# Waits for attention and for the next unit's bank moved ahead of the last feed-forward matmuls

## Chip, cores and metric

One core of one Trainium2 chip. The metric is device time in microseconds (us) of one execution; the median over several executions is compared.

## What is computed

Three stages follow each other on 4 x 576 tokens of width 512 (8 heads of 64). The parts that matter here, cut from the reference:

```python
# 1: windowed attention; heads 0-3 see 32 keys back, heads 4-7 see every 4th of 128
scores = np.where(masks, scale * q @ k.T, -1e9)
attn = softmax(scores) @ v
# 2: token-shifted feed-forward
xk = mu_k * x + (1 - mu_k) * x_prev ; xr = mu_r * x + (1 - mu_r) * x_prev
k = np.maximum(xk @ w_k, 0.0)
x = sigmoid(xr @ w_r) * (k * k @ w_v)
# 3: low-rank mix over tokens, then a second feed-forward
u = x + (x.T @ U @ V).T
out = u + np.maximum(u @ w_ch1, 0.0) @ w_ch2
```

## The kernel before, in words

It is written by hand: each engine has its own program, and the order of work on an engine is the order of its text. Engines wait for each other with counting semaphores; the helper `wait` (L366) puts a wait in front of the next instruction of the engine. TensorE (PE) runs its queue in order, so everything behind an unmet wait stands still.

**Feed-forward units.** Stage 2 goes over the tokens in 9 chunks of 256 (`NC1`, the PE function `chunk`, L1274). A chunk has 10 units in the order of `UNITS` (L148): eight "k" units (one 128-column block of `xk @ w_k`) and two "r" units (`xr @ w_r`). A unit is 4 steps over the contraction, each a call of `three` (L1185), which issues three fp32r matmuls (high x high, low x high, high x low), so 12 matmuls: 256 moving columns in a k unit, 512 in an r unit. Units alternate between two PSUM banks (`unit_bank`). ScalarE (ACT) empties a bank (`relu_k`, L843, or `sig`, L849) and counts `unit_out`; before writing, unit n waits until unit n-2 was emptied. After some units come the matmuls of `k*k @ w_v` for the blocks named in `V_AFTER` (L149), six of 512 columns for each block; these wait for `sql_done`, which VectorE (DVE) counts at L1050.

**Attention visits.** Attention of the tokens that later chunks need is woven in between. It works on 32 pieces (8 parts k of the tokens times 4 pairs of heads p), each in four steps: A transposes q and k, B makes scores, C transposes the probabilities, D multiplies with v. `SLOT_OF` gives each step a place behind one of the 10 units; what stands behind a unit is called its visit here. From chunk 1 on the visits behind units 0, 3, 5 and 8 hold an A and a C step, those behind units 1, 4, 6 and 9 a B and a D step; units 2 and 7 have none. On PE `other_work` (L1245) runs them: after the unit and its w_v matmuls, except behind unit 9, where the visit stands ahead of these. The A steps and C steps are transposes (L1203, L1205, L1232), the B and D steps small matmuls into 64-column halves of the array (L1226, L1241).

Every step writes one or two of four banks that are used in turn. In `attention` (L1191) PE waits, bank by bank, until the bank's last use was emptied; A also waits for its q and k loads, B until its A was copied out, C for the normalised probabilities (`normed`, DVE L1023), D for its v load and until its C was copied out. ACT copies C's banks out at L733 (`probs_t`), in the order of its own program: after the unit's relu and square, the first half of the exponentials of the B step in the visit before (L743), then A's `q_t` copy (L724), then `probs_t`. Its counter is `att_scalar`, that of DVE's copies `att_vector`.

```python
                    if GROUP[key] >= ABANKS:
                        wait_drained(pe, GROUPS[GROUP[key] - ABANKS])
                    ...
                        pe.wait_ge(values_in[n % VALUES], V_COUNT[n])
                        wait_drained(pe, last_bank("C", k, p))
```

Chunks 7 and 8 carry the token mix of stage 3 in place of attention; from 418 us on the second feed-forward runs alone.

Of the kernel before, what the change touches and what calls it, by code (L numbers as in the profile page):

```python
# [30 lines left out]
D = H * DH  # L31
# [8 lines left out]
KT = D // P  # L40
# [54 lines left out]
def steps_in(slot):  # L95
    return sorted([step for step, n in SLOT_OF.items() if n == slot], key=lambda step: ("ACBD".index(step[0]), step[1:]))
# [26 lines left out]
def last_bank(st, k, p):  # L123
    return (st, k, p, banks_of((st, k, p)) - 1)
# [84 lines left out]
def build(nc, q, k_in, v, mu_k, mu_r, w_k, w_v, w_r, u_in, v_in, w_ch1, w_ch2, out):  # L209
    ctx = ExitStack()  # L210
    with ctx:
# [159 lines left out]
        def wait(eng, s, value):  # L371

            value = value + CREDIT.get(id(s), 0)
            if isinstance(value, int) and value <= 0:
                return
            eng.wait_ge(s, value)

        def wait_drained(eng, key):

            n = GROUP[key]  # L380
            if drained_by_scalar(key):
                wait(eng, att_scalar, SCALAR_N[n])
            else:
                wait(eng, att_vector, VECTOR_N[n])

        def wait_mm(eng, key):

# [794 lines left out]
        def _(pe):  # L1182
            pe.sem_inc(o_mm, CREDIT[id(o_mm)])

            def three(dst, lhs, rhs, start, stop):  # L1185
# [2 lines left out]
                pe.matmul(dst, lhs[0], rhs[1], start=False, stop=False)  # L1188
                return pe.matmul(dst, lhs[1], rhs[0], start=False, stop=stop)  # L1189

            def attention(stage_, k, p):  # L1191
                n, dil, half = nth(k, p), DILATED[p], k % 2
                for j in range(banks_of((stage_, k, p))):
                    key = (stage_, k, p, j)
                    dst = abank(key)
                    if GROUP[key] >= ABANKS:
                        wait_drained(pe, GROUPS[GROUP[key] - ABANKS])
                    if stage_ == "A":
                        if j == 0:
                            pe.wait_ge(qk_in[n % RAWS], QK_COUNT[n])  # L1200
                        raw = (q_raw, k_raw)[j][n % RAWS]
                        for t in range(2):
                            ins = pe.transpose(dst[:, t * P:t * P + P], raw[:, t, :], ident[:, :])  # L1203
                        if half:
                            ins = pe.transpose(dst[:, WHOLE:WHOLE + TAIL], raw[0:TAIL, 2, :], ident[0:TAIL, 0:TAIL])  # L1205
                    elif stage_ == "B":
                        if j == 0:
                            wait_drained(pe, ("A", k, p, 0))
                            wait_drained(pe, ("A", k, p, 1))
                        every = units(k, p)  # L1210
                        for i, (query, col, keys) in enumerate(every):
                            if (i == DILATION and dil) != (j == 1):
                                continue
                            if not dil:
                                rhs = k_t[p][:, FROM[half] + UQ * i:FROM[half] + UQ * i + keys]
                            elif keys == 2 * UK:
                                rhs = k_t[p][:, 0:S].rearrange("p (r j) -> p r j", r=DILATION)[:, :, SUB - UK // 2:SUB]
                            else:
                                first_key = SUB * i + (JCUT - WINDOW if half else 0)
                                rhs = k_t[p][:, first_key:first_key + keys]  # L1220
                            col -= every[DILATION][1] if j else 0
                            for h in range(2):
                                out_ = dst[DH * h:DH * h + DH, col:col + keys]
                                if keys == 2 * UK:
                                    out_ = out_.rearrange("p (r j) -> p r j", r=DILATION)
                                ins = pe.matmul(out_, q_t[n % 2][:, h, query:query + UQ], rhs, start=True, stop=True)  # L1226
                    elif stage_ == "C":
                        if j == 0:
                            wait(pe, normed, n + 1)
                        cols = [(col + UK * a, min(keys, UK)) for _, col, keys in units(k, p) for a in range(max(1, keys // UK))]  # L1230
                        for i, (col, keys) in enumerate(cols[4 * j:4 * j + 4]):
                            ins = pe.transpose(dst[0:keys, i * P:i * P + P], probs[n % 2][:, col:col + keys], ident[:, :])  # L1232
                    else:
                        pe.wait_ge(values_in[n % VALUES], V_COUNT[n])
                        wait_drained(pe, last_bank("C", k, p))
                        for i, (query, _, keys) in enumerate(units(k, p)):
                            blocks = max(1, keys // UK)
                            for a in range(blocks):
                                for h in range(2):
                                    rows, kk = slice(DH * h, DH * h + DH), min(keys, UK)  # L1240
                                    ins = pe.matmul(dst[rows, query:query + UQ], v_raw[n % VALUES][0:kk, i + a, rows],  # L1241
                                                    probs_t[n % 2][0:kk, i + a, rows], start=a == 0, stop=a == blocks - 1)
                    ins.then_inc(att_mm, 1)

            def other_work(c, n):  # L1245

                if c < MIX_CHUNK:
                    for step in steps_in(c * NUNIT + n):
                        attention(*step)
                else:  # L1250
                    for step in mix_steps("tensor", [(c - MIX_CHUNK) * NUNIT + n]):
                        mix_step(*step)

            def turn(c, t):
# [16 lines left out]
                                       x[:, n, t * P:t * P + P] if start else u_tile[:, t, n * P:n * P + P], ident[:, :])  # L1271
                ins.then_inc(t_mm, 1)

            def chunk(c):  # L1274
                last = c == NC1 - 1
                for n, (kind, m) in enumerate(UNITS):
                    wait(pe, unit_out, c * NUNIT + n - 1)
                    dst = unit_bank[n % 2]
                    if kind == "k":
                        if m == 0:  # L1280
                            wait(pe, xkl_done, c + 1)
                        if c == 0 and m % 2 == 0:
                            pe.wait_ge(w_split, SPLIT1["k", m // 2])
                        cols = slice((m % 2) * P, (m % 2) * P + P)
                        for t in range(KT):
                            ins = three(dst[:, 0:C1], (wk_h[:, m // 2, t, cols], wk_l[:, m // 2, t, cols]),
                                        (xs_h[:, 0, t, :], xs_l[:, 0, t, :]), t == 0, t == KT - 1)
                    else:
                        if m == 0:
                            wait(pe, xrl_done, c + 1)  # L1290
                        if c == 0 and m == 0:
                            pe.wait_ge(w_split, SPLIT1["r", 1])
                        cols = slice(m * P, m * P + P)
                        for t in range(KT):
                            ins = three(dst[:, :], (xs_h[:, 1, t, cols], xs_l[:, 1, t, cols]),
                                        (wr_h[:, t, :], wr_l[:, t, :]), t == 0, t == KT - 1)
                    ins.then_inc(unit_mm, 1)
                    if last and n == NUNIT - 1:
                        for t in range(T2):
                            turn(0, t)  # L1300
                    if n == NUNIT - 1:
                        other_work(c, n)
                    for m2 in V_AFTER[n]:
                        if m2 == 0:
                            wait(pe, x2_done, c * T1)
                        if c == 0 and m2 % 2 == 0:
                            pe.wait_ge(w_split, SPLIT1["v", m2 // 2])
                        wait(pe, sql_done, c * M1 + m2 + 1)
                        for t in range(T1):
                            cols = slice(t * P, t * P + P)  # L1310
                            ins = three(v_bank[t][:, :], (sq_h[:, m2 % KRING, cols], sq_l[:, m2 % KRING, cols]),
                                        (wv_h[:, m2, :], wv_l[:, m2, :]), m2 == 0, m2 == M1 - 1)
                        ins.then_inc(v_mm, 1)
                    if n < NUNIT - 1:
                        other_work(c, n)
# [35 lines left out]
            pe.wait_ge(consts, 1)  # L1351
            pe.wait_ge(cleared, 3)
            for step in BEFORE:
                attention(*step)
            for c in range(NC1):
                chunk(c)
# [65 lines left out]
```

## Time and profile before

| | |
|---|---|
| time, median of 3 | 834.91 us (834.12 to 838.01) |
| profiled execution: its own time | 836.28 us |
| its span, first to last instruction | 834.5 us |
| PE busy in the span | 794.1 us (95%) |
| DVE busy | 323.6 us (39%) |
| ACT busy | 332.2 us (40%) |
| GpSimd (POOL) busy | 152.1 us (18%) |
| mean granted PE clock | 0.977 |

The profile is one execution. The timeline gives start and duration of each instruction, equal ones merged. PE's durations are modelled and overlap, so the distance between two starts says how long a matmul holds the engine. "PEld" is the weight load of a matmul. A bracket at a row's end is the engine's idle time before it and what ended it; the list of waits sums these up.

### The profile page before, as it was taken

What the parts mean: (1) busy time and instruction counts of PE and PEld (TensorE: products, weight loads), DVE (VectorE), ACT (ScalarE), POOL (GpSimd) and SP (SyncE); (2) the same over time, 40 slices, a digit from 0 to 9 for tenths busy, and PEclk for the clock granted to TensorE, in tenths of its full rate; (3) what the DMA queues carried; (4) which work ended last, traced back from release to release, by engine and by line L of the source; (5) the groups of instructions that cost most, each with busy time, mean ns of one, the idle gap of its engine ahead of it and who ended that gap; (6) DMA issues with size and microseconds to landing.
All of it is one profiled execution on the core that took longest, in us unless ns stands there. A gap on an engine that the chain in (4) does not pass through costs nothing.

```text
span 834.5 us, 13588 instructions
## 1 busy us (share of the span) xinstructions
PE 794.1 (95%) x5176; PEld 695.9 (83%) x5176; DVE 323.6 (39%) x660; ACT 332.2 (40%) x885; POOL 152.1 (18%) x169
## 2 busy tenths in 40 slices
PE   5579999989999999989999999999999999999998
PEld 4357888878888888877889899999989999999997
DVE  5556846464647463673541131121122113113111
ACT  5558676767676765552343211111111111111110
POOL 5694201030102012330056500000000000000000
PEclk8679999999999999998999999999999999999999
DMA  5544231023212200100023210000000000001001
GB/s 130 145 125 114 63 82 45 14 74 83 55 42 59 55 14 1 51 7 20 1 95 132 77 39 1 1 25 12 0 0 38 0 0 38 0 0 38 1 0 38
DMA packets 83349, 35.78 MB, mean 43 GB/s; under 512 B 71136, under 2 KB 77280, under 8 KB 83296
## 3 DMA queue, kind: packets, MB, share of 16 engines
q1 hardware_dynamic: 83296, 35.07, 15.3%
q8 instruction: 33, 0.54, 0.3%
q14 instruction: 20, 0.16, 0.1%
HBM read 30.33 MB, written 4.72 MB: 42 GB/s over the span
## 4 chain that ended last, share of the span: by engine, by line
PE 86%; DVE 4%; ACT 3%; POOL 2%; SPq 2%; issue 1%; DMA 1%; DVEq 0%; ACTq 0%; POOLq 0%
PE bank L1187 25%; PE bank L1189 25%; PE bank L1188 25%; PE bank L1226 3%; PE bank L1232 2%; PE bank L1241 2%; PE bank L1203 2%; SPq L449 1%; PE bank L1270 1%; DMA k_raw<-in_k_dram 1%; PE bank L1205 1%; DVE sq L1046 1%; PE bank L1329 1%; ACT probs L743 1%; POOL wr_l L622 1%
## 5 line engine op out<-in xcount | busy, mean ns | idle before, releaser
L925 ACT ACTIVATE h_h<-bank 128x384 fp32r<-128x384 f32 x96 | 47.2, 492 | 332.2 <-PE bank L1189 332.2
L1157 DVE SCALAR_TENSOR_TENSOR h_l<-bank,h_h 128x384 fp32r<-128x384 f32 x96 | 53.5, 557 | 308.9 <-ACT h_h L925 308.9
L1187 PE MATMUL bank<-ut_h,w_h 128*128 128x384 f32 x384 | 130.4, 340 | 0.0
L1189 PE MATMUL bank<-ut_h,w_l 128*128 128x384 f32 x384 | 129.3, 337 | 0.0
L1188 PE MATMUL bank<-ut_l,w_h 128*128 128x384 f32 x384 | 128.9, 336 | 0.0
L1189 PE MATMUL bank<-w_h,h_l 128*128 128x512 f32 x288 | 113.8, 395 | 0.0
L1188 PE MATMUL bank<-w_l,h_h 128*128 128x512 f32 x288 | 113.6, 394 | 0.0
L1187 PE MATMUL bank<-w_h,h_h 128*128 128x512 f32 x288 | 112.0, 389 | 0.0
L1187 PE MATMUL bank<-xs_h,wk_h 128*128 128x256 f32 x288 | 85.9, 298 | 0.7 <-DVE xs_l L1116 0.7
L1188 PE MATMUL bank<-xs_l,wk_h 128*128 128x256 f32 x288 | 81.6, 283 | 0.0
L1189 PE MATMUL bank<-xs_h,wk_l 128*128 128x256 f32 x288 | 81.4, 283 | 0.0
L1187 PEld LDWEIGHTS bank<-ut_h,w_h 128*128 128x128 f32 x384 | 72.2, 188 | 3.1
L1188 PEld LDWEIGHTS bank<-ut_l,w_h 128*128 128x128 f32 x384 | 72.2, 188 | 3.1
L1189 PEld LDWEIGHTS bank<-ut_h,w_l 128*128 128x128 f32 x384 | 72.1, 188 | 0.0
L843 ACT ACTIVATE relu_k<-bank 128x256 f32<-128x256 f32 x72 | 27.2, 377 | 102.4 <-PE bank L1189 101.8
L1187 PE MATMUL bank<-wv_h,sq_h 128*128 128x512 f32 x144 | 58.9, 409 | 6.1 <-DVE sq_l L1050 6.1
L1189 PEld LDWEIGHTS bank<-w_h,h_l 128*128 128x128 f32 x288 | 54.0, 188 | 11.5
L1188 PEld LDWEIGHTS bank<-w_l,h_h 128*128 128x128 f32 x288 | 54.0, 188 | 9.4
L1187 PEld LDWEIGHTS bank<-w_h,h_h 128*128 128x128 f32 x288 | 54.1, 188 | 8.9
L1187 PEld LDWEIGHTS bank<-xs_h,wk_h 128*128 128x128 f32 x288 | 55.4, 192 | 4.6 <-DVE xs_l L1116 1.4
L1188 PE MATMUL bank<-wv_l,sq_h 128*128 128x512 f32 x144 | 57.4, 399 | 0.0
L1189 PE MATMUL bank<-wv_h,sq_l 128*128 128x512 f32 x144 | 57.4, 399 | 0.0
(126 smaller groups left out, 1341.3 us busy)
## 6 DMA issues: line engine op xcount, KB each, us to landing
stage<-in_moe_w_ch_dram SPq DMA_DIRECT2D x16, 512.0 KB, 3.3
out_dram<-result SPq DMA_DIRECT2D x18, 256.0 KB, 2.0
q_raw<-in_q_dram SPq DMA_DIRECT2D x64, 64.0 KB, 2.2
k_raw<-in_k_dram SPq DMA_DIRECT2D x64, 64.0 KB, 2.2
v_raw<-in_v_dram SPq DMA_DIRECT2D x32, 64.0 KB, 2.3
stage<-in_moe_w_k_dram SPq DMA_DIRECT2D x4, 512.0 KB, 4.2
stage<-in_moe_w_v_dram SPq DMA_DIRECT2D x4, 512.0 KB, 3.8
v_raw<-in_v_dram SPq DMA_DIRECT2D x16, 96.0 KB, 2.6
```

The costliest lines, as they stand in the source:

```text
L449: sp.dma_start(dst[:, 0:2, DH * h:DH * h + DH], rows.rearrange("(t p) d -> p t d", p=P)).then_inc(landed, 16)
L622: ins = pool.tensor_tensor(lo[:, a], raw[:, a], hi[:, a].bitcast(F32), ALU.subtract)
L843: act.activation(relu_k[:, m % 2, :], unit_bank[n % 2][:, 0:C1], ACT.Relu).then_inc(unit_out, 1)
L925: act.activation(h_h[:, m % KRING, :], h_bank[m % 2][:, 0:C2], ACT.Relu).then_inc(hh_done, 1)
L1157: dve.scalar_tensor_tensor(h_l[:, m % KRING, :], h_bank[m % 2][:, 0:C2], 0.0, h_h[:, m % KRING, :].bitcast(F32), op0=ALU.max, op1=ALU.subt ...
L1187: pe.matmul(dst, lhs[0], rhs[0], start=start, stop=False)
L1188: pe.matmul(dst, lhs[0], rhs[1], start=False, stop=False)
L1189: return pe.matmul(dst, lhs[1], rhs[0], start=False, stop=stop)
L1203: ins = pe.transpose(dst[:, t * P:t * P + P], raw[:, t, :], ident[:, :])
L1226: ins = pe.matmul(out_, q_t[n % 2][:, h, query:query + UQ], rhs, start=True, stop=True)
L1232: ins = pe.transpose(dst[0:keys, i * P:i * P + P], probs[n % 2][:, col:col + keys], ident[:, :])
L1241: ins = pe.matmul(dst[rows, query:query + UQ], v_raw[n % VALUES][0:kk, i + a, rows], probs_t[n % 2][0:kk, i + a, rows], start=a == 0, stop ...
```

## The change

`attention` on PE loses all its waits. The new `attention_waits` issues, for all steps of a visit together, the waits for their banks, loads, copies and normalised probabilities. In the part before the chunks and in chunk 0 it is called right ahead of each step. In chunks 1 to 6 the new `ahead` calls it inside the unit, before the fourth call of `three`, or, where w_v matmuls stand between the unit and its visit, before the last call of `three` of those. `ahead` also takes the wait for `unit_out` that the next unit needs to the same place, in all nine chunks. No compute instruction is added, taken away or put elsewhere.

```diff
@@ -383,6 +383,15 @@
             else:
                 wait(eng, att_vector, VECTOR_N[n])
 
+        def wait_all_drained(eng, keys):
+
+            by_scalar = [SCALAR_N[GROUP[key]] for key in keys if drained_by_scalar(key)]
+            by_vector = [VECTOR_N[GROUP[key]] for key in keys if not drained_by_scalar(key)]
+            if by_scalar:
+                wait(eng, att_scalar, max(by_scalar))
+            if by_vector:
+                wait(eng, att_vector, max(by_vector))
+
         def wait_mm(eng, key):
 
             wait(eng, att_mm, GROUP[key] + 1)
@@ -1188,25 +1197,34 @@
                 pe.matmul(dst, lhs[0], rhs[1], start=False, stop=False)
                 return pe.matmul(dst, lhs[1], rhs[0], start=False, stop=stop)
 
+            def attention_waits(steps):
+
+                keys = [GROUPS[GROUP[st, k, p, j] - ABANKS] for st, k, p in steps for j in range(banks_of((st, k, p)))
+                        if GROUP[st, k, p, j] >= ABANKS]
+                keys += [("A", k, p, j) for st, k, p in steps if st == "B" for j in range(2)]
+                keys += [last_bank("C", k, p) for st, k, p in steps if st == "D"]
+                wait_all_drained(pe, keys)
+                for st, k, p in steps:
+                    n = nth(k, p)
+                    if st == "A":
+                        pe.wait_ge(qk_in[n % RAWS], QK_COUNT[n])
+                    elif st == "C":
+                        wait(pe, normed, n + 1)
+                    elif st == "D":
+                        pe.wait_ge(values_in[n % VALUES], V_COUNT[n])
+
             def attention(stage_, k, p):
                 n, dil, half = nth(k, p), DILATED[p], k % 2
                 for j in range(banks_of((stage_, k, p))):
                     key = (stage_, k, p, j)
                     dst = abank(key)
-                    if GROUP[key] >= ABANKS:
-                        wait_drained(pe, GROUPS[GROUP[key] - ABANKS])
                     if stage_ == "A":
-                        if j == 0:
-                            pe.wait_ge(qk_in[n % RAWS], QK_COUNT[n])
                         raw = (q_raw, k_raw)[j][n % RAWS]
                         for t in range(2):
                             ins = pe.transpose(dst[:, t * P:t * P + P], raw[:, t, :], ident[:, :])
                         if half:
                             ins = pe.transpose(dst[:, WHOLE:WHOLE + TAIL], raw[0:TAIL, 2, :], ident[0:TAIL, 0:TAIL])
                     elif stage_ == "B":
-                        if j == 0:
-                            wait_drained(pe, ("A", k, p, 0))
-                            wait_drained(pe, ("A", k, p, 1))
                         every = units(k, p)
                         for i, (query, col, keys) in enumerate(every):
                             if (i == DILATION and dil) != (j == 1):
@@ -1225,14 +1243,10 @@
                                     out_ = out_.rearrange("p (r j) -> p r j", r=DILATION)
                                 ins = pe.matmul(out_, q_t[n % 2][:, h, query:query + UQ], rhs, start=True, stop=True)
                     elif stage_ == "C":
-                        if j == 0:
-                            wait(pe, normed, n + 1)
                         cols = [(col + UK * a, min(keys, UK)) for _, col, keys in units(k, p) for a in range(max(1, keys // UK))]
                         for i, (col, keys) in enumerate(cols[4 * j:4 * j + 4]):
                             ins = pe.transpose(dst[0:keys, i * P:i * P + P], probs[n % 2][:, col:col + keys], ident[:, :])
                     else:
-                        pe.wait_ge(values_in[n % VALUES], V_COUNT[n])
-                        wait_drained(pe, last_bank("C", k, p))
                         for i, (query, _, keys) in enumerate(units(k, p)):
                             blocks = max(1, keys // UK)
                             for a in range(blocks):
@@ -1246,6 +1260,8 @@
 
                 if c < MIX_CHUNK:
                     for step in steps_in(c * NUNIT + n):
+                        if c == 0:
+                            attention_waits([step])
                         attention(*step)
                 else:
                     for step in mix_steps("tensor", [(c - MIX_CHUNK) * NUNIT + n]):
@@ -1271,10 +1287,19 @@
                                        x[:, n, t * P:t * P + P] if start else u_tile[:, t, n * P:n * P + P], ident[:, :])
                 ins.then_inc(t_mm, 1)
 
+            def ahead(c, n):
+
+                if 1 <= c < MIX_CHUNK and steps_in(c * NUNIT + n):
+                    attention_waits(steps_in(c * NUNIT + n))
+                if n < NUNIT - 1:
+                    wait(pe, unit_out, c * NUNIT + n)
+
             def chunk(c):
                 last = c == NC1 - 1
                 for n, (kind, m) in enumerate(UNITS):
-                    wait(pe, unit_out, c * NUNIT + n - 1)
+                    visit_after_unit = n == NUNIT - 1 or not V_AFTER[n]
+                    if n == 0:
+                        wait(pe, unit_out, c * NUNIT - 1)
                     dst = unit_bank[n % 2]
                     if kind == "k":
                         if m == 0:
@@ -1283,6 +1308,8 @@
                             pe.wait_ge(w_split, SPLIT1["k", m // 2])
                         cols = slice((m % 2) * P, (m % 2) * P + P)
                         for t in range(KT):
+                            if t == KT - 1 and visit_after_unit:
+                                ahead(c, n)
                             ins = three(dst[:, 0:C1], (wk_h[:, m // 2, t, cols], wk_l[:, m // 2, t, cols]),
                                         (xs_h[:, 0, t, :], xs_l[:, 0, t, :]), t == 0, t == KT - 1)
                     else:
@@ -1292,6 +1319,8 @@
                             pe.wait_ge(w_split, SPLIT1["r", 1])
                         cols = slice(m * P, m * P + P)
                         for t in range(KT):
+                            if t == KT - 1 and visit_after_unit:
+                                ahead(c, n)
                             ins = three(dst[:, :], (xs_h[:, 1, t, cols], xs_l[:, 1, t, cols]),
                                         (wr_h[:, t, :], wr_l[:, t, :]), t == 0, t == KT - 1)
                     ins.then_inc(unit_mm, 1)
@@ -1308,6 +1337,8 @@
                         wait(pe, sql_done, c * M1 + m2 + 1)
                         for t in range(T1):
                             cols = slice(t * P, t * P + P)
+                            if t == T1 - 1 and m2 == V_AFTER[n][-1] and not visit_after_unit:
+                                ahead(c, n)
                             ins = three(v_bank[t][:, :], (sq_h[:, m2 % KRING, cols], sq_l[:, m2 % KRING, cols]),
                                         (wv_h[:, m2, :], wv_l[:, m2, :]), m2 == 0, m2 == M1 - 1)
                         ins.then_inc(v_mm, 1)
@@ -1351,6 +1382,7 @@
             pe.wait_ge(consts, 1)
             pe.wait_ge(cleared, 3)
             for step in BEFORE:
+                attention_waits([step])
                 attention(*step)
             for c in range(NC1):
                 chunk(c)
```

Two places show how the waits move on PE, in chunk 5. Lines L1187 to L1189 of before are L1196 to L1198 of the change, and L1226 and L1241 are L1244 and L1255. Names of semaphores stand behind "waits".

First, unit 1 and its visit, a B and a D step, before:

```order
L1187 MATMUL bank1<-xs_h,wk_h 128x256
L1188 MATMUL bank1<-xs_l,wk_h 128x256
L1189 MATMUL bank1<-xs_h,wk_l 128x256
L1226 MATMUL bank4<-k_t3,q_t1 64x96 [waits att_vector,att_scalar]
L1226 MATMUL bank4<-k_t3,q_t1 64x96 x7
L1241 MATMUL bank5<-probs_t1,v_raw1 64x64 [waits att_scalar,values_in1]
L1241 MATMUL bank5<-probs_t1,v_raw1 64x64 x7
L1187 MATMUL bank0<-xs_h,wk_h 128x256 [waits unit_out]
```

and with the change:

```order
L1196 MATMUL bank1<-xs_h,wk_h 128x256 [waits values_in1,unit_out,att_vector,att_scalar]
L1197 MATMUL bank1<-xs_l,wk_h 128x256
L1198 MATMUL bank1<-xs_h,wk_l 128x256
L1244 MATMUL bank4<-k_t3,q_t1 64x96 x8
L1255 MATMUL bank5<-probs_t1,v_raw1 64x64 x8
L1196 MATMUL bank0<-xs_h,wk_h 128x256
```

All waits of the visit (v load, both copies) and that of unit 2 for its bank now stand three matmuls ahead of the visit; the B and D steps and unit 2 begin without a wait.

Second, the w_v matmuls behind unit 5 and the visit with an A and a C step, before:

```order
L1187 MATMUL bank3<-wv_h,sq_h 128x512
L1188 MATMUL bank3<-wv_l,sq_h 128x512
L1189 MATMUL bank3<-wv_h,sq_l 128x512
L1203 MATMUL bank4<-ident,q_raw2 128x128 [waits qk_in2,att_scalar]
L1203 MATMUL bank4<-ident,q_raw2 128x128
L1205 MATMUL bank4<-ident,q_raw2 128x64
L1203 MATMUL bank5<-ident,k_raw2 128x128 [waits att_vector]
L1203 MATMUL bank5<-ident,k_raw2 128x128
L1205 MATMUL bank5<-ident,k_raw2 128x64
L1232 MATMUL bank6<-ident,probs1 96x128 [waits normed,att_vector]
L1232 MATMUL bank6<-ident,probs1 96x128 x3
L1187 MATMUL bank0<-xs_h,wk_h 128x256 [waits unit_out]
```

and with the change:

```order
L1196 MATMUL bank3<-wv_h,sq_h 128x512 [waits normed,qk_in2,unit_out,att_vector,att_scalar]
L1197 MATMUL bank3<-wv_l,sq_h 128x512
L1198 MATMUL bank3<-wv_h,sq_l 128x512
L1224 MATMUL bank4<-ident,q_raw2 128x128 x2
L1226 MATMUL bank4<-ident,q_raw2 128x64
L1224 MATMUL bank5<-ident,k_raw2 128x128 x2
L1226 MATMUL bank5<-ident,k_raw2 128x64
L1248 MATMUL bank6<-ident,probs1 96x128 x4
L1196 MATMUL bank0<-xs_h,wk_h 128x256
```

The wait for `normed`, which stood ahead of the C step's first transpose, is now ahead of the last three w_v matmuls, together with the load's and the banks'. Where no w_v matmuls follow a unit, as with units 1, 6 and 9, the waits stand inside the unit as in the first place.

## Rows read from the trace of the kernel before

**Rows 1.** Waits of PE, 95.2 to 336.6 us: total, times, longest.

```profile
PE bank L1187 <- DVE sq_l L1050: 2.2, 5, 0.8
PE bank L1203 <- DMA k_raw<-in_k_dram: 1.4, 1, 1.4
```

**Rows 2.** Waits of PE, 95.2 to 420 us (all chunks from 1 on).

```profile
PE bank L1187 <- DVE sq_l L1050: 5.8, 6, 3.7
```

**Rows 3.** Waits of ACT, 95.2 to 336.6 us.

```profile
ACT relu_k L843 <- PE bank L1189: 62.2, 16, 6.5
```

**Rows 4.** Timeline of PE: start, us, instruction; where hoisted waits will stand.

```profile
243.96 0.28 PE L1187 MATMUL bank<-xs_h,wk_h 128*128 128x256 f32 x1
...
253.60 0.28 PE L1187 MATMUL bank<-xs_h,wk_h 128*128 128x256 f32 x1
...
263.61 0.28 PE L1187 MATMUL bank<-xs_h,wk_h 128*128 128x256 f32 x1
...
280.99 0.40 PE L1187 MATMUL bank<-wv_h,sq_h 128*128 128x512 f32 x1
...
284.31 0.28 PE L1187 MATMUL bank<-xs_h,wk_h 128*128 128x256 f32 x1
...
294.93 0.28 PE L1187 MATMUL bank<-xs_h,wk_h 128*128 128x256 f32 x1
...
306.25 0.28 PE L1187 MATMUL bank<-xs_h,wk_h 128*128 128x256 f32 x1
...
306.69 0.55 PE L1226 MATMUL bank<-k_t,q_t 128*64 128x96 f32 x8
...
339.09 0.28 PE L1187 MATMUL bank<-xs_h,wk_h 128*128 128x256 f32 x1
```

**Rows 5.** Timeline of ACT: the C step's copies for the six visits.

```profile
244.31 0.76 ACT L733 ACTIVATE probs_t<-bank 96x512 f32<-96x512 f32 x2
...
253.52 0.59 ACT L733 ACTIVATE probs_t<-bank 64x512 f32<-64x512 f32 x1
...
264.11 0.59 ACT L733 ACTIVATE probs_t<-bank 64x512 f32<-64x512 f32 x1
...
284.38 0.59 ACT L733 ACTIVATE probs_t<-bank 96x512 f32<-96x512 f32 x1
...
295.12 0.86 ACT L733 ACTIVATE probs_t<-bank 96x512 f32<-96x512 f32 x2
...
305.95 0.87 ACT L733 ACTIVATE probs_t<-bank 96x512 f32<-96x512 f32 x2
```

**Rows 6.** Timeline of DVE: the normalising that C waits for, chunk 5.

```profile
280.53 0.56 DVE L1023 TENSOR_TENSOR probs<-probs,inv 128x384 f32<-128x384 f32 x1
```

**Rows 7.** Timeline of ACT: the relu that frees a unit bank, chunk 7.

```profile
338.24 0.39 ACT L843 ACTIVATE relu_k<-bank 128x256 f32<-128x256 f32 x1 [2.87 <-PE bank L1189]
```

**Rows 8.** Timeline of PE: the visit in chunk 3 whose load is late.

```profile
180.24 0.41 PE L1203 MATMUL bank<-ident,q_raw 128*128 128x128 f32 x2 [1.44 <-DMA k_raw<-in_k_dram]
```

**Rows 9.** Timeline of PE: first matmuls after a wait that was not met.

```profile
300.50 0.50 PE L1187 MATMUL bank<-wv_h,sq_h 128*128 128x512 f32 x1 [0.39 <-DVE sq_l L1050]
300.84 0.39 PE L1188 MATMUL bank<-wv_l,sq_h 128*128 128x512 f32 x1
301.07 0.40 PE L1189 MATMUL bank<-wv_h,sq_l 128*128 128x512 f32 x1
```

**Rows 10.** Timeline of PE: unit 3 begins behind two met waits.

```profile
309.77 0.29 PE L1189 MATMUL bank<-xs_h,wk_l 128*128 128x256 f32 x1
309.89 0.40 PE L1187 MATMUL bank<-wr_h,xs_h 128*128 128x512 f32 x1
```

**Rows 11.** Timeline of PEld: load of a 64-row transpose, no wait.

```profile
303.72 0.14 PEld L1205 LDWEIGHTS bank<-ident,q_raw 64*128 64x128 f32 x1 [0.16 <-issue]
```

**Rows 12.** Timeline of PE: unit 2 begins behind a D step.

```profile
308.36 0.39 PE L1187 MATMUL bank<-xs_h,wk_h 128*128 128x256 f32 x1
308.59 0.28 PE L1188 MATMUL bank<-xs_l,wk_h 128*128 128x256 f32 x1
```

## The prediction

> **What bounds the kernel now.** I read the share of busy time first: PE works 794 of 834.5 us (95%, in the table above), no other engine passes 40%. So anything that makes PE stand still is paid in full unless it takes the place of an idle time that is there already. The list of waits says how much of that there is. In chunks 1 to 6, where the moved waits stand, PE waits 2.2 us for `sql_done` (five times) and 1.4 us for one load [rows 1]; no wait of an attention visit on a copy or on `normed` is in the list. Up to the end of chunk 8 the waits for `sql_done` come to 5.8 us, the longest 3.7 [rows 2]. In the same stretch ACT waits for PE 62.2 us, but in only 16 pieces [rows 3]: it has room on average and runs behind PE in bursts. In those bursts, at the new place of each wait, the question is whether what is waited for has happened. That is read from the timeline, engine beside engine.
>
> **The change, part by part.** It adds and removes no compute instruction. It moves the waits of the visits in chunks 1 to 6, and all waits for a unit's bank, three matmuls ahead: 3 x 0.12 us in a k unit (309.77 to 309.89 is one pitch [rows 10]), 3 x 0.23 where w_v matmuls stand there (300.84 to 301.07 [rows 9]). It also draws the D step's wait, which stood behind the B step, to the same place. Behind the waiting matmul everything on PE is queued: the rest of the unit, the visit, the next unit; and ACT and DVE wait for the unit's end.
>
> *Visits with B and D.* D needs the copy of the C step of the visit just before. Behind units 0 and 5 and 8 follows one k unit, and nine of its matmuls (1.05 us) are all that now lies between that C step and the wait. The ends of the copies, start plus duration [rows 5], against the starts of the matmul that will carry the wait [rows 4]:
> chunk 5, behind unit 1: 264.70 against 263.61, 1.09 late;
> chunk 5, unit 6: 284.97 against 284.31, 0.66;
> chunk 5, unit 9: 295.98 against 294.93, 1.05;
> chunk 6, unit 1: 306.82 against 306.25, 0.57;
> chunk 4, unit 6: 245.07 against 243.96, 1.11;
> chunk 4, unit 9: 254.11 against 253.60, 0.51.
> The plan of visits repeats every two chunks, so these are six kinds. They occur 2, 3, 3, 3, 2 and 2 times in chunks 1 to 6 (in chunk 3 the late load gives ACT time before unit 1, and the last pieces in chunk 6 are thin): 2.2 + 2.0 + 3.2 + 1.7 + 2.2 + 1.0 = **12.3 us**. The visits behind unit 4 have a whole r unit of room and are met.
>
> *Visits with A and C.* `normed` is ready at 281.09 [rows 6] against 280.99 [rows 4]: 0.1 late, in three odd chunks, **0.3**. The other visits of this kind are met.
>
> *The late load.* In chunk 3 PE idles 1.44 us for k today [rows 8]. The idle stays, but ahead of three more matmuls: **0.35**. In that visit ACT now gets the unit's relu and square only after the idle, so the next B and D visit loses its cover and should look like its kind: 1.1 more.
>
> *Restart.* Behind an unmet wait PE's second matmul comes 0.34 us after the first where 0.23 is usual [rows 9], 0.1 more. From the producer's end to PE's first matmul lies between nothing and one pitch of 0.12; I take 0.1. With 19 unmet waits that were not there, 0.2 each: **3.8**. Gross: 12.3 + 0.3 + 0.35 + 1.1 + 3.8 = 17.9.
>
> *Given back.* Where two late visits follow each other (behind units 5 and 6 in odd chunks) the first stall of 0.3 lets ACT come nearer: 0.9. The waits for `sql_done` at chunk ends close chains over ACT and DVE that a standing PE shortens; between nothing and all of 2.2 us [rows 1] I take all, since ACT is the late one in each of them as in the visits. The 3.7 us in chunk 7 [rows 2] I leave as it is: by then ACT has waited for PE again. **Net: 17.9 - 0.9 - 2.2 = 14.8 us.**
>
> *Bank waits of units.* The smallest margin I find is in chunk 7: the relu ends at 338.63 [rows 7], the wait will stand at 339.09 [rows 4]. Met, 0. If one in ten of the 80 were late by 0.1, 0.8. In chunk 0 and before, waits only join the first bank of their own step, behind the wait for that step's operand: 0, at most 0.5.
>
> *What met waits may give back.* This is what speaks for the change. The 23 visits with B and D (four a chunk, three in chunk 6) begin late: the first starts at 306.69, where 306.25 [rows 4] plus three pitches of 0.12, 306.60, was due: 0.09 x 23 = 2.0 us. Behind the D step the first two matmuls of the unit are 0.23 apart where 0.12 is usual [rows 12], 0.11, and I allow as much again for the start itself: 4.9 us. So the gain lies between 0 and 6.9. I take 0. Unit 3 begins behind two met waits with the usual pitch of 0.12 [rows 10], so a met wait costs nothing; and a 64-row transpose with no wait at all has its weight load idle for 0.16 [rows 11], so it is the change of the array's tile that costs, and it stays. The Trainium skill, "TensorEngine Tiling (Array Packing)", section Tiling Modes, states that a switch of the tiling mode drains the engine; by that rule the gain is nothing and the sum stays, and the row agrees. For the change speaks the Trainium skill, "TensorE: Matmul & The Clock Gate", section Part 3: Packing small matmuls: TensorE's queue pulls weight loads ahead of matmuls in flight. Were a wait what stops it at these places, the sum would be 6.9 us smaller by that rule; no row here shows that.
>
> The profiled execution took 836.3 us, 1.8 more than its span and 1.4 more than the median of 834.9. 836.3 + 14.8 = 851.1; against the median, **849.7 us**, 1.8% slower. A measurement of this kernel can tell about 0.5% (4.2 us) from no change.
>
> **The rivals.**
> *Weight loads freed (slower, but less).* All 23 entries and exits lose their gap: 14.8 - 6.9 = 7.9, 842.8 us. For it: every late entry does carry a wait. Against it: [rows 10, 11].
> *ACT in step after one stall (the other side).* ACT's 62.2 us of waiting [rows 3] show that it could keep up. If its lateness is a fixed backlog and not a distance from PE's visits, the first stall (1.1 + 0.2) and the moved idle (0.35) put PE behind it for good and later waits are met: 1.7 us lost, 836.6 us, no change. With the 6.9 us from the loads on top it is 5.2 us faster, 829.7. It decides at ACT's copy behind unit 1 of chunk 2: if that follows PE's transposes by the same time as now, the stall recurs. Against it: the C copy waits for C's transposes of the visit just before, which PE issues after its own stall, and 16 rejoinings in six chunks mean that the backlog is made anew each time.
> *No relief.* Nothing is given back, and the unit banks and chunk 0 cost their bounds: 17.9 + 1.3 = 19.2, 854.1 us.
>
> **How the numbers follow.** Forecast 0.63; loads freed 0.14; no relief 0.08; in step without the loads 0.07 (no change); in step with them 0.08 (faster). Slower by over 0.5%: 0.63 + 0.14 + 0.08 = 0.85; within: 0.07; faster: 0.08. The range takes in the three slower cases and leaves out the two others: 841.5 to 855 us. The forecast's own range is 847 to 853.
>
> **What would show it.** In the new list of waits PE should have waits on ACT's `probs_t`, some 15 of them, 0.5 to 1.3 us each, ahead of the fourth group of units 1, 6 and 9, and `normed` three times at 0.1 to 0.3; chunks 1 to 6 should take 14 to 16 us more than their 241.4, all after them the same. PE's busy time should stay. The first L1244 of a visit should still start 0.2 us after the unit's last matmul. I am wrong if those waits are missing, if they shrink from chunk to chunk, or if entry and exit gaps close.

## The result and the profile after

| | before | with the change |
|---|---|---|
| time, median | 836.25 us (4 runs) | 848.12 us (846.69 to 848.71, 4 runs) |
| ratio | | 1.0142, 95% interval 1.0115 to 1.0168 |
| span of the profiled execution | 834.5 us | 846.4 us |
| PE busy | 794.1 us (95%) | 799.8 us (94%) |
| PE waits for ACT's `probs_t` at L1187 / L1196 | none | 8.1 us, 12 in the list |

The kernel became slower by 11.9 us. Forecast were 849.7 us and a range of 841.5 to 855. The spans split it. By the start of each chunk's first matmul in both traces, chunk 1 begins at 95.17 us before and 94.23 after; chunks 1 to 6 take 241.5 and 255.3 us; chunks 7 and 8 take 81.4 and 80.5; all after that takes 416.4 in both. So the stretch that holds the moved waits lost 13.8 us, and 0.9 each came back at the start and in chunk 7.

The windows view of the changed kernel (start and end, length, busy time of PE, PEld, DVE, ACT and POOL, then granted clock, DMA share and GB/s) gives the stretch of chunks 1 to 6, and a short one in it:

```profile
94.20:349.50 255.30, 243.01 (x2051) 204.71 (x2050) 138.90 (x326) 169.14 (x499) 38.91 (x50) 0.99 0.20 45
183.90:187.10 3.20, 3.18 (x15) 3.06 (x16) 1.18 (x3) 2.11 (x8) 0.00 (x0) 0.50 0.35 80
```

The same count of PE instructions as before (2051) takes 255.3 us in place of 241.4. ACT and DVE do the same work as before. Where PE stands is in the list of its waits, for the same stretch, against [rows 1]:

```profile
PE bank L1196 <- ACT probs_t L742: 8.1, 12, 1.0
PE bank L1196 <- issue: 2.0, 1, 2.0
PE bank L1196 <- DVE sq_l L1059: 1.2, 3, 0.4
PE bank L1196 <- DVE probs L1032: 0.6, 3, 0.2
```

The first and last rows are new: copies of the C step and `normed`. The second is the late load of chunk 3, now ahead of the unit's last matmuls. `sql_done` fell from 2.2 to 1.2 us. ACT now waits more often for PE, against [rows 3]:

```profile
ACT relu_k L852 <- PE bank L1198: 76.6, 31, 8.4
```

One stall beside its cause. The timeline of PE in chunk 5, inside unit 1 (start, duration, instruction; in brackets the idle time before it):

```profile
272.78 0.27 PE L1198 MATMUL bank<-xs_h,wk_l 128*128 128x256 f32 x1
274.03 0.39 PE L1196 MATMUL bank<-xs_h,wk_h 128*128 128x256 f32 x1 [0.98 <-ACT probs_t L742]
274.25 0.28 PE L1197 MATMUL bank<-xs_l,wk_h 128*128 128x256 f32 x1
274.37 0.28 PE L1198 MATMUL bank<-xs_h,wk_l 128*128 128x256 f32 x1
274.58 0.46 PE L1244 MATMUL bank<-k_t,q_t 128*64 128x96 f32 x5
```

and that of ACT at the same time:

```profile
273.39 0.59 ACT L742 ACTIVATE probs_t<-bank 64x512 f32<-64x512 f32 x1
```

The copy ends at 273.98 and PE goes on at 274.03. The unit's fourth group starts 1.25 us after the third's last matmul where 0.12 is usual: 1.13 lost, and 0.1 more since the second matmul comes 0.22 after the first. Forecast for this place were 1.09 late and 0.2 for the restart, 1.29 against 1.23. The entry into the visit keeps its gap: 274.37 to 274.58 is 0.21 us, though no wait stands there any more.

### The profile page after: what moved, and what is told of

The parts are those of the page before. It is cut to its first block, busy times and chain, and to the rows that moved or that the text cites. A ratio compares the mean times of both kernels' runs of the same rounds, so it can differ in the third digit from the quotient of the medians.

```text
span 846.4 us, 13574 instructions
## 1 busy us (share of the span) xinstructions
PE 799.8 (94%) x5176; PEld 697.7 (82%) x5176; DVE 326.0 (39%) x660; ACT 332.8 (39%) x885; POOL 151.9 (18%) x169
## 4 chain that ended last, share of the span: by engine, by line
PE 83%; ACT 6%; DVE 5%; issue 3%; POOL 1%; SPq 1%; DMA 1%; DVEq 0%; ACTq 0%; POOLq 0%
PE bank L1196 25%; PE bank L1198 24%; PE bank L1197 24%; PE bank L1244 3%; PE bank L1255 2%; ACT probs L752 1%; ACT q_t L733 1%; PE bank L1248 1%; PE bank L1224 1%; ACT probs_t L742 1%; PE bank L1286 1%; ACT L752 1%; DVE sq L1055 1%; DVE sq_l L1059 1%; PE bank L1360 1%
## 5 line engine op out<-in xcount | busy, mean ns | idle before, releaser
L1196 PE MATMUL bank<-ut_h,w_h 128*128 128x384 f32 x384 | 130.4, 340 | 0.0
L1198 PE MATMUL bank<-ut_h,w_l 128*128 128x384 f32 x384 | 129.3, 337 | 0.0
L1198 PE MATMUL bank<-w_h,h_l 128*128 128x512 f32 x288 | 113.7, 395 | 0.0
L1196 PE MATMUL bank<-w_h,h_h 128*128 128x512 f32 x288 | 111.9, 389 | 0.0
L1196 PE MATMUL bank<-xs_h,wk_h 128*128 128x256 f32 x288 | 88.7, 308 | 11.6 <-ACT probs_t L742 8.1
L1198 PE MATMUL bank<-xs_h,wk_l 128*128 128x256 f32 x288 | 82.2, 286 | 0.0
L1196 PEld LDWEIGHTS bank<-ut_h,w_h 128*128 128x128 f32 x384 | 72.2, 188 | 3.2
L1198 PEld LDWEIGHTS bank<-ut_h,w_l 128*128 128x128 f32 x384 | 72.0, 188 | 0.0
L1196 PEld LDWEIGHTS bank<-xs_h,wk_h 128*128 128x128 f32 x288 | 56.3, 195 | 18.7 <-ACT probs_t L742 11.5
L1196 PE MATMUL bank<-wv_h,sq_h 128*128 128x512 f32 x144 | 58.5, 406 | 5.7 <-DVE sq_l L1059 5.1
L1198 PEld LDWEIGHTS bank<-w_h,h_l 128*128 128x128 f32 x288 | 54.0, 187 | 11.5
L1196 PEld LDWEIGHTS bank<-w_h,h_h 128*128 128x128 f32 x288 | 54.1, 188 | 9.0
L1197 PEld LDWEIGHTS bank<-xs_l,wk_h 128*128 128x128 f32 x288 | 56.4, 196 | 1.3
L1198 PE MATMUL bank<-wv_h,sq_l 128*128 128x512 f32 x144 | 57.1, 397 | 0.0
```

The costliest lines, as they stand in the source:

```text
L1196: pe.matmul(dst, lhs[0], rhs[0], start=start, stop=False)
```

## Experiments

Two theories stood. Theory 1, by which the forecast was made: a moved wait costs as much as its event is late at the new place, and nothing when it is met. Theory 2: waits inside a row of matmuls break the stream, whatever their state. A third reading, that a met wait at the head of a visit or unit holds back the weight load, was the change's chance of a gain. The medians of before lay between 834.80 and 836.25 us (836.25 is that of the table above, from four runs; the others rest on 14 to 23 runs and lie at 834.80 to 835.03, against which the change's 848.12 is 13 us more); each ratio is against the runs of before that were timed together with the experiment. The diffs are shortened; those of e5, e8 and e9 are made to the kernel before, all others to the change.

### e1: joined, not moved

```diff
 def ahead(c, n):
-    if 1 <= c < MIX_CHUNK and steps_in(c * NUNIT + n):
-        attention_waits(steps_in(c * NUNIT + n))
-    if n < NUNIT - 1:
-        wait(pe, unit_out, c * NUNIT + n)
+    pass
 def other_work(c, n):
+    if c >= 1 and steps_in(c * NUNIT + n):
+        attention_waits(steps_in(c * NUNIT + n))
 def chunk(c):
-    if n == 0:
-        wait(pe, unit_out, c * NUNIT - 1)
+    wait(pe, unit_out, c * NUNIT + n - 1)
```

> A visit's waits are issued together, but right at the visit's start, and the wait for a unit's bank is where it was before: the joining without the moving ahead. Theory 1 (a moved wait costs by how late its event is at the new place): each of the 15 late copies is 0.35 us less late than in the change, so 0.74, 0.31, 0.70, 0.22, 0.76 and 0.16 us in the six kinds, 7.0 us in all, 1.5 for restarts, less about 1.5 given back: 6 to 8 us over the kernel before. Theory 2 (waits inside a unit's row of matmuls break its stream, whatever their state): 0 to 1 us over before.

Measured: 840.84 us, before 834.80; ratio 1.0067 (1.0039 to 1.0095). That is 6.0 us more, and chunks 1 to 6 took 248.6 us, 7.1 more than before. PE's waits in that stretch:

```profile
PE bank L1244 <- ACT probs_t L742: 4.3, 10, 0.6
PE bank L1224 <- DMA k_raw<-in_k_dram: 2.6, 1, 2.6
PE bank L1196 <- DVE sq_l L1059: 1.8, 4, 0.6
```

Joining alone draws the D step's copy ahead of the B step, which used to cover it. Not all of the 7.1 us is of that kind, though. In chunk 3 the stall for k was 2.93 us from start to start where it was 1.72 before, and behind it the granted clock fell to its lower level, which cost another 1.5 us by the distances. The windows view of that stretch:

```profile
183.40:186.80 3.40, 3.40 (x23) 3.18 (x22) 1.07 (x3) 2.18 (x9) 0.00 (x0) 0.50 0.42 93
```

What is left for the joining is about 4.5 us, a third of the 13.8 us that the change lost in these chunks, with no wait moved into a unit. That the median fell into the 6 to 8 us of theory 1 is in part luck: by its own terms the theory came out too high here.

### e2: the D step's waits stay with D

```diff
 def ahead(c, n):
-    attention_waits(steps_in(c * NUNIT + n))
+    attention_waits([step for step in steps_in(c * NUNIT + n) if step[0] != "D"])
 def other_work(c, n):
-    if c == 0:
+    if c == 0 or step[0] == "D":
         attention_waits([step])
```

> As the change, but the D step's waits (its C copy, its bank, its load) stay right ahead of D. Theory 1: the copy that remains ahead of the unit's end is that of q_t, which ends 0.48 us (unit 1, odd chunks), 0.33 (unit 6, even), 0.16 and 0.04 us late or is met; with normed 0.1 x 3, restarts and the late load it comes to 3 to 5.5 us over before. Theory 2: nearly as many waits stand inside units as in the change, so 9 to 12 us over before.

Measured: 839.32 us, before 834.80; ratio 1.0048 (1.0030 to 1.0067), 4.5 us more. The list of PE's waits in chunks 1 to 6:

```profile
PE bank L1196 <- issue: 2.3, 1, 2.3
PE bank L1196 <- DVE sq_l L1059: 2.0, 5, 0.7
PE bank L1196 <- ACT q_t L733: 1.5, 5, 0.4
PE bank L1196 <- DVE probs L1032: 0.6, 3, 0.2
```

`probs_t` is gone from it; what is left is the earlier copy, `q_t`, and `normed`. With the D step's waits ahead of D again, some two thirds of the change's loss are gone (chunks 1 to 6 took 245.6 us, 4.2 more than before, of which 0.9 is a longer stall for the load). Theory 2 expected 9 us or more.

### e3: only the unit banks' waits ahead

```diff
 def ahead(c, n):
-    if 1 <= c < MIX_CHUNK and steps_in(c * NUNIT + n):
-        attention_waits(steps_in(c * NUNIT + n))
     if n < NUNIT - 1:
         wait(pe, unit_out, c * NUNIT + n)
 def other_work(c, n):
-    if c == 0:
-        attention_waits([step])
+    attention_waits([step])
```

> Only the wait for the next unit's bank is moved ahead, in all nine chunks; the visits' waits stand ahead of their step. Theory 1: these are met with 0.46 us or more to spare, so -1 to +1 us against before. Theory 2: 80 waits inside units at some 0.1 us: 5 to 8 us over before. Theory 3 (a met wait at a unit's start holds back the weight load behind a D step): the exits close, 0.2 us x 23, 4 to 5 us under before.

Measured: 835.50 us, before 834.80; ratio 1.0002 (0.9989 to 1.0016). Some 80 met waits inside units cost nothing, and taking them away from the heads of units gains nothing. Chunks 1 to 6 take 241.4 us, as before. Theory 2 and the third reading are both out for these waits.

### e4: six matmuls ahead in place of three

```diff
-    if t == KT - 1 and visit_after_unit:
+    if t == KT - 2 and visit_after_unit:
         ahead(c, n)
-    if t == T1 - 1 and m2 == V_AFTER[n][-1] and not visit_after_unit:
+    if t == 0 and m2 == V_AFTER[n][-1] and not visit_after_unit:
         ahead(c, n)
```

The first of the two stands in the loops of the k and of the r units alike.

> As the change, but all moved waits stand six matmuls ahead of the unit's end in place of three. Theory 1: each of the 15 late copies is 0.35 us later still, 5.3 us, normed and one or two more copies become late: 18 to 22 us over before, 6 to 9 over the change. Theory 2: the same number of waits inside units, so as the change within 1 us.

Measured: 855.98 us, before 834.80; ratio 1.0250 (1.0217 to 1.0284), 21.2 us more, and about 8 more than the change. PE's waits in chunks 1 to 6:

```profile
PE bank L1196 <- ACT probs_t L742: 11.3, 13, 1.3
PE bank L1196 <- DVE probs L1032: 2.8, 4, 0.9
...
PE bank L1196 <- ACT relu_k L852: 1.0, 2, 0.5
```

The copies are 3.2 us worse, `normed` 2.2, and the first unit banks are late too. With the distance alone changed, the loss moves as theory 1 says (18 to 22 us over before were expected). The load's stall and a fall of the clock behind it are in chunk 3 of both e4 and the change.

### e5 and e6: one DMA moved, PIECE_V

```diff
 if n == nth(3, 0):
     load_piece(PIECE_U)
+if n == nth(3, 3):
     load_piece(PIECE_V)
```

In e5 this is done to the kernel before, in e6 to the change.

> The kernel before with one 72 KB x 4 weight load of the token mix (PIECE_V) issued three pairs later on the DMA queue, so that the load of chunk 3 that is late is not behind it. The 1.44 us of idle time of PE in chunk 3 go, and nothing else changes: 1 to 2 us under before on either theory.

> The change with the same move of PIECE_V. The changed kernel spends 3.8 us more around its late load than an undisturbed chunk (2.2 us of stall and some 1.2 us in which the granted clock is at its lower level and 0.35 of matmuls). Theory 1: these go, but the copy behind unit 1 of chunk 3 is then late like its kind, 1.14 us and 0.1 for the restart, which it was not in the change: 2 to 3.2 us under the change, 8.5 to 10.5 over before. If that visit were not late, 3.5 to 4 under the change.

Measured: e5 834.58 us against 834.85, ratio 0.9998 (0.9981 to 1.0016); e6 849.28, ratio 1.0171 (1.0136 to 1.0205). Both misses. I had taken the wrong transfer: PE's idle in chunk 3 was still there in e5,

```profile
PE bank L1204 <- DMA k_raw<-in_k_dram: 1.6, 1, 1.6
```

and the DMA queue of e5 issues another piece, a `w_ch` load, right behind the end of GpSimd's split:

```profile
173.17 0.37 SPq L497 DMA_DIRECT2D stage<-in_moe_w_ch_dram  x1
173.58 1.19 SPq L465 DMA_DIRECT2D v_raw<-in_v_dram  x2
174.82 1.12 SPq L449 DMA_DIRECT2D q_raw<-in_q_dram  x2
175.98 0.98 SPq L449 DMA_DIRECT2D k_raw<-in_k_dram  x2
```

```profile
172.28 0.87 POOL L669 TENSOR_TENSOR u_split<-stage,u_split 128x320 fp32r<-128x320 f32 x1
```

That load (FIRST2) waits for the split, and v, q and k stand behind it in the queue. In e6 the stall stayed as well, but PE's clock did not fall behind it (granted 1.00 where the change has 0.50), 1.6 us less; and behind unit 1 of chunk 3 a stall of 1.15 us appeared that the change does not have. Chunks 1 to 6 so take 254.7 us, 0.6 less than in the change; its span is 0.9 us longer than the change's all the same, for what lies ahead of chunk 1 and in chunk 7, as is told below.

### e7 and e8: ScalarE's copies ahead of its exponentials

```diff
 def attention_slot(slot):
-    for k, p in behind: exps(k, p, 0)
     for step in steps_in(slot): attention(*step)
+    for k, p in behind: exps(k, p, 0)
     for k, p in behind: exps(k, p, 1)
```

In e7 this is done to the change, in e8 to the kernel before; both halves of the exponentials stand behind the copies.

> The change, with ScalarE's copies of a visit (q_t, probs_t) ahead of both halves of the exponentials, not between them. If the copies are late because they stand behind that work in ScalarE's queue, the stalls behind unit 6 (1.14 x 2, 0.27 x 3) and unit 1 of even chunks (0.61 x 3) vanish and those of unit 1 in odd chunks halve (1.14 x 2), while those of unit 9, which have no exponentials in front, stay (0.84 x 3, 0.6 x 2): 5 to 8 us under the change, 4 to 7 over before. If they are late by PE's distance alone, no change against the change.

> The kernel before with the same order on ScalarE. PE waits for no copy there but for 0.27 us twice and 0.13 us twice, which go: 0 to 1.5 us under before.

Measured: e7 847.70 us against 834.85, ratio 1.0152 (1.0128 to 1.0176), no better than the change where 5 to 8 us were expected; e8 838.94, ratio 1.0056 (1.0033 to 1.0079), 4.1 us worse where a small gain was expected. Both times miss. What came true is that the copies came earlier: PE's waits for `probs_t` in e7 fell from 12 to 8,

```profile
PE bank L1195 <- ACT probs_t L742: 5.7, 8, 1.1
...
PE bank L1195 <- DVE probs L1034: 1.2, 3, 0.4
...
PE bank L1195 <- ACT relu_k L851: 0.6, 3, 0.2
```

and between the two traces the stalls of unit 6 in even chunks went from 1.14 us to 0.05, those of unit 1 in even chunks from 0.61 to 0, in odd chunks from 1.14 to 0.43. But the 2 us of exponentials and table load now run later, and the relu of the next unit behind them: new stalls came in odd chunks around unit 8 (0.36 for its bank, 0.15 to 0.2 for `sql_done`, 0.56 for `normed`) and those of unit 9 grew by 0.2 to 0.7. So behind units 1 and 6 it is ACT's queue, not a transfer or DVE, that makes the copies late, and reordering it gains nothing: what goes first makes something else late within the same chunk. In e8 it is the same: PE loses 0.6 us for `sql_done` behind unit 8 in odd chunks and 0.4 to 0.7 ahead of the B step behind unit 9 in chunks 1 to 5, and the stall for k is 0.6 longer. Behind unit 9 no exponentials stand in front of the copy, and what makes it late there was not tested.

### e9 and e10: the right DMA moved, FIRST2

```diff
-if n == nth(4, 0):
+if n == nth(5, 0):
     load_piece(FIRST2)
```

> The kernel before, with the first weight load of the second feed-forward (FIRST2) issued four pairs later, ahead of part 5 in place of part 4. In the trace of before that load is issued at 174.62 us, right behind GpSimd's last u_split at 174.59, and the k load that PE waits for stands behind it in the DMA queue. If that is the cause, PE's idle of 1.4 to 2 us in chunk 3 goes: 1 to 2 us under before.

> The change with the same move of FIRST2. The stall of 2.17 us, its restart and the stretch at the lower granted clock (1.2 us) go. Theory 1: the copy behind unit 1 of chunk 3 is then late like its kind, about 1.2 us: 1.5 to 2.7 us under the change, 9 to 11 over before. If it is not late, 3 to 4 under the change.

Measured: e9 833.55 us against 835.03, ratio 0.9984 (0.9971 to 0.9996), 1.5 us less. The wait for k is gone from PE's list in chunks 1 to 6, which is now one row:

```profile
PE bank L1187 <- DVE sq_l L1050: 2.1, 5, 0.8
```

e10: 845.07, ratio 1.0121 (1.0099 to 1.0144), 10.0 us over before and 3.0 under the change (2.7 in chunks 1 to 6). With the load in time, the copy behind unit 1 of chunk 3 is late like its kind. The timeline of PE in e10:

```profile
183.37 0.27 PE L1198 MATMUL bank<-xs_h,wk_l 128*128 128x256 f32 x1
184.63 0.39 PE L1196 MATMUL bank<-xs_h,wk_h 128*128 128x256 f32 x1 [0.98 <-ACT probs_t L742]
```

1.26 us from start to start, the same as in chunk 5 of the change. With the load in time in both kernels, the moved waits cost 11.5 us by the medians of e9 and e10 and 12.7 us in chunks 1 to 6, so the loss does not hang on the late load.

### e11: only the met waits ahead

On top of e9; of the change only this part:

```diff
 def ahead(c, n):
+    early = [step for step in steps_in(c * NUNIT + n) if step[0] == "A"] if 1 <= c < MIX_CHUNK else []
+    if early:
+        attention_waits(early)
     if n < NUNIT - 1:
         wait(pe, unit_out, c * NUNIT + n)
 def other_work(c, n):
+    if c == 0 or step[0] != "A":
         attention_waits([step])
```

> FIRST2 later as in e9; of the waits only those that are met at the new place are moved ahead: those of the A steps and those for a unit's bank; B, C and D steps wait right ahead of themselves. Theory 1, by which a met wait costs nothing wherever it stands: as e9 within 1 us. If a met wait at a visit's or a unit's start holds up weight loads, 2 to 5 us under e9.

Measured: 833.29 us against 835.03, ratio 0.9969 (0.9953 to 0.9985). Against e9's 833.55 that is 0.3 us less, and chunks 1 to 6 take 239.6 us where e9 takes 239.9; these runs cannot tell either from nothing. e9 and e11 are the fastest versions, 1.5 and 1.7 us under before; what they gain is the load in time.

## Why the prediction was right

**The copies of the C step** were the main term: 12.3 us for the lateness in 15 places, and restarts. They came at 15 places, 10.9 us by the distances from start to start in both traces (what of the restart lies ahead of the first matmul included; the list of waits has 12 of the places and leaves out three with an idle time of 0.11 or 0.12), and another 1.6 for the second matmuls. By kind, lateness as forecast and time lost at the first matmul: unit 1 in odd chunks 1.09 and 1.14; unit 6 in even ones 1.11 and 1.14; unit 1 in even ones 0.57 and 0.61; unit 9 in even ones 0.51 and 0.58. These came as forecast; the two other kinds, both in odd chunks, came smaller (next point).

**Given back** was mis-sized in its parts. Behind a first stall in odd chunks I expected 0.3 us of relief at unit 6 only. Unit 6 lost 0.27 in place of 0.66, and unit 9, where I had counted none, 0.84 in place of 1.05. From `sql_done` I took back all 2.2 us of [rows 1]; 1.2 came. The two errors stand on opposite sides. There came 0.8 that I had not counted: in chunks 2 and 4 the D step had lost 0.29 to the same copy at its own place, and in chunks 1 and 5 the B step behind unit 1 had begun 0.13 late.

**The restart** was sized at 0.2; the rows show 0.05 from the copy's end to the start and 0.1 for the second matmul.

**The late load.** I expected 0.35, and 1.1 with restart for the visit behind it, whose cover would go. In the change the stall grew by 0.6 us, and the visit behind was not late. Something else took that place: the clock. After an idle of 2.0 us [second row of the waits after] the granted clock was 0.50, its lower level of 1.2 GHz, for 3.2 us [windows row above]; the 15 PE instructions in them took 1.6 us longer by their distances than in e6, where the clock stayed. In that time ACT caught up. e6 and e10, without the fall, show the 1.15 us stall that I had forecast. So the term is right where PE runs at 2.4 GHz. In the change it was wrong, and that a cost of much the same size stood in its place, which I had not seen, is luck.

**`normed`** was late three times, as forecast: 0.1 each and the restart; the distances grew by 0.36 and 0.07, together 1.3 for 0.9. **Unit banks**: nothing, shown by e3.

**Met waits.** I took 0 of a possible 6.9 us, because [rows 10, 11] showed a met wait at no cost and a tile change without a wait at 0.16. After the change the entry into a B step is still 0.21 us, and the exit from a D step the same as in [rows 12]:

```profile
321.23 0.38 PE L1196 MATMUL bank<-xs_h,wk_h 128*128 128x256 f32 x1
321.45 0.28 PE L1197 MATMUL bank<-xs_l,wk_h 128*128 128x256 f32 x1
```

The gap belongs to the switch of tile, with or without a wait. (The second sum of the 6.9 us, 0.22 x 23, is 5.1 and not 4.9; as the term was taken at 0, nothing hangs on it.) The Trainium skill, "TensorEngine Tiling (Array Packing)", section Tiling Modes, states that a switch of the tiling mode drains the engine; these rows agree.

**The rivals.** Loads freed: out, by the rows above, e3 and e11. ACT in step after one stall: out; a stall of 1.14 us in chunk 1 recurs in chunk 5, 0.98 of it idle both times. It holds in part inside a chunk, as the relief shows; that ACT's 31 waits for PE are what ends it is argued, not tested. No relief: 854.1 is 6 us too high.

The sum for chunks 1 to 6 was 14.8 us and 13.8 came. By the spans the whole change cost 11.9: another 0.9 us is missing since chunk 1 began earlier, and 0.9 since the clock's fall behind the stall of chunk 7 (3.7 us in [rows 2]), which stands in every trace, set in 1.1 us after it where before it set in at once. That the median still lies only 1.6 under the forecast is in part luck: I had taken off 1.4 us because the profiled execution of before lay above its median, and in the change the two are the same (848.2 and 848.12). Neither of the 0.9 can be put down to the change. The start of chunk 1 lay between 93.7 and 95.2 us in all thirteen traces, whose kernels are nearly the same up to there. And e6, e7 and e10, which have the change's code in chunk 7, show the early fall, while e8, which has that of before, shows the later one.

## What to carry to other kernels

Before moving a wait ahead, read from the timeline when its event happens at the new place: the difference, times the number of places, is the main part of the price (12.3 us were forecast here, and 10.9 came at the first matmuls), and the second matmul adds 0.1 at each place. A wait that is met cost nothing at either place here (e3, e11), so there was nothing to gain from moving it. Joining the waits of several steps to one place takes the cover of the earlier steps away from the later ones; here that alone was a third of the loss. If a transfer is late, look for the instruction that was issued at the moment when its queue went on, and for what that one had waited for.

## What was unexpected of the hardware

PE's granted clock fell to 1.2 GHz behind the change's stall in chunk 3 (2.28 us from start to start) and stayed there for 3.2 us, at a cost of 1.6 us. The length of the stall does not tell when that happens. Behind the stall for the same load it also fell in e1 (2.93 us) and e4 (2.12, the fall 1.3 us after its end). Before (1.72), e5 and e7 (1.92), e3 (1.97) and e6 (2.03) kept the clock, but so did e8, whose stall is as long as the change's (2.28), and e2, whose is longer (2.59). The stretch behind it in e8:

```profile
181.00:184.20 3.20, 3.17 (x36) 2.99 (x36) 1.18 (x3) 2.62 (x11) 0.00 (x0) 1.00 0.27 59
```

And the stall of chunk 7, 4.06 us in all thirteen traces, is followed by the fall at once in seven (the next two starts 0.59 or 0.60 and 0.43 us apart) and 0.4 to 1.1 us later in six (in the change 0.34 and 0.23). What decides is left open. The price of one stall so differs by 1 to 1.6 us between runs of nearly the same program, as much as e9 gained.
